# The first MLP's leaky ReLU on three engines, without the linear product, and its output product three slots behind

## The chip, the cores and the metric

One NeuronCore of a Trainium2 chip runs the kernel. The metric is the device time of one execution in microseconds (us).

## The reference

All sizes and steps, with x running through one attention and two MLPs:

```python
# attention: q (12288 x 128), kv pooled 4x4 to 768 keys, then @ w_sr; k = v
s = (q @ k.T) / sqrt(128); a = exp(s - max); a /= a.sum() + 1e-9; x = a @ v
# first MLP: 128 -> 2048 -> 128
h = x @ w_in;  g = maximum(0.01 * h, h);  x = g @ w_out
# second MLP: 128 -> 2048 -> 128
h = x @ w_in2; g = where(h >= 1, h, where(h <= -1, 0, (h + 1)**2 / 4)); out = g @ w_out2
```

## The kernel before

The 12,288 tokens are cut into 24 blocks of 512 (TB). Everything is kept transposed: channels on the partitions, tokens along the free axis. The hidden 2,048 channels of each MLP are 16 chunks (FC) of 128, one per slot `s`.

Every matmul operand is split into a high part (fp32r) and the low part that is left, so each product is three matmuls of 512 columns: low weight with high data, high weight with high data, high weight with low data (`product`, L484 to L488). This is why each intermediate needs a high part (a copy, by ScalarE) and a low part (a subtraction, by VectorE or GpSimd).

Each engine has its own program, and semaphores tie them together. All programs go through iterations `j`, each of 16 slots. Iteration j works on three blocks at once: the first MLP of block j, the second MLP of block j-1 (and the last chunks of block j-2), and the attention of block j+1. Iteration 0 has no second MLP, iteration 23 has no attention, iteration 24 has the second MLP alone. Before iteration 0 stand the pooling of kv, the splitting of the weights and block 0's attention.

Names used below, with the line where each is issued:

- `mlp1_in(s)`: the hidden product of the first MLP, chunk s, into one of two PSUM banks `h1`. It waits until the chunk two back has been read. `mlp1_out(s)`: the output product of chunk s, added up in `sum1`; it is issued LAG1 slots behind.
- `mlp2_in(s)`, `mlp2_out(s)`: the same of the second MLP (`h2`, `sum2`), LAG2 = 3 slots behind.
- g1 high: ScalarE, L342, a ReLU from PSUM. g1 low: VectorE, L458, `max(h, 0) - high`.
- ramp: ScalarE, L351, into `g2`. bend: VectorE, L445, `min(g2, 1) * g2`, both inputs in SBUF. above: VectorE, L451, `max(h, g2)`. g2_high: ScalarE, L329. g2_low: GpSimd, L267.
- attention of the next block: `score` (4 of them, slots 0, 2, 4, 6), row maximum (L377), exponential (L283, slots 1, 3, 5, 7), normalisation (L288, slots 2, 4, 6, 8), transposes (L507, slots 9 to 14) with high and low part (L293, L390), `values` (slots 10 to 15), attended high and low part (L297, L395).
- x2 high and low part (L369, L477): the first MLP's sum as input of the second.

The leaky ReLU is written as a sum: `max(0.01 h, h) = 0.99 (relu(h) + h * 0.01 / 0.99)`. The second term is linear in x, so its path through both weights is one 128 x 128 matrix `lin`, made once before iteration 0 from 16 matmuls (L553), and applied to the block by one product at slot 2 of each iteration, ahead of the first `mlp1_out`:

```python
def mlp1_out(s):
    fs = slice(s * P, (s + 1) * P)
    if s == 0:
        product(sum1, lin_hi[:], lin_lo[:], x_hi[:], x_lo[:], True, False)
    pe.wait_ge(g1_split, j * FC + s + 1)
```

GpSimd's queue, in order: the identity, the low part of the queries, the split of w1_out, four quarters of w1_in's low part (each waits for ScalarE, which does the second to fourth inside slots 0 to 2 of iteration 0), the splits of w2_in and w2_out, and then its iterations.

The lines that a program prints:

## Time and profile before

| | |
|---|---|
| device time, median of 3 runs | 1396.45 us (1395.6 to 1396.55) |
| the profiled execution's span, first to last instruction | 1394.2 us |
| TensorE busy | 1368.8 us, 98% of the span |
| VectorE busy | 1035.5 us, 74% |
| ScalarE busy | 950.9 us, 68% |
| GpSimd busy | 563.7 us, 40% |

The trace gives the span; the execution's own time around it is not recorded apart, and the median of the runs is 2.3 us above the span. Times in the trace count from the span's start. A matmul's row lasts longer than the distance to the next, since matmuls overlap; distances between starts tell the pace. A row's time before the engine's name is its start, then its duration. Where a row ends in brackets, the engine sat idle that long, until the operation named there was done.

### The profile page before, as it was taken

Reading aid. Unit: us, or ns where it says so; the run is one execution under the profiler, and the core shown is the slowest. Engines: PE = TensorE matmul, PEld = TensorE weight load, DVE = VectorE, ACT = ScalarE, POOL = GpSimd, SP = SyncE. Lnnn points to the kernel's source line nnn. Section 1 sums busy time; section 2 is a strip of 40 time slices with the busy share of each in tenths; the row PEclk is TensorE's granted clock in tenths of the full one; section 3 lists DMA queues with packets and bytes.
Section 4 is the critical chain, followed back from the end, with each engine's and each line's share of the span. In section 5 each row is a group of like instructions: output and inputs, shape, how many; then the busy total and the mean of one; then the engine's idle time right before and its main releaser. Section 6 shows DMA issues by size and latency. Waiting matters only on the chain.

```text
span 1394.2 us, 21088 instructions
## 1 busy us (share of the span) xinstructions
PE 1368.8 (98%) x6320; PEld 1115.3 (80%) x6320; DVE 1035.5 (74%) x1660; ACT 950.9 (68%) x1695; POOL 563.7 (40%) x424
## 2 busy tenths in 40 slices
PE   5999999999999999999999999999999999999997
PEld 4788888888888888888888888888888888888884
DVE  6577777777777777777787777777877777777777
ACT  3676776766767667677676676776766767667665
POOL 2534344334334344343434434344334334344346
PEclk9999999999999999999999999999999999999999
DMA  8000000000000000000000000000000000000000
GB/s 348 16 0 8 9 15 8 8 15 8 8 8 8 15 8 8 15 2 13 8 8 15 8 8 8 8 15 8 8 15 8 8 8 8 15 0 9 8 1 16
DMA packets 9525, 24.44 MB, mean 18 GB/s; under 512 B 1057, under 2 KB 1185, under 8 KB 8865
## 3 DMA queue, kind: packets, MB, share of 16 engines
q1 hardware_dynamic: 9504, 24.19, 4.9%
q8 instruction: 11, 0.18, 0.1%
q14 instruction: 10, 0.07, 0.0%
HBM read 17.89 MB, written 6.29 MB: 17 GB/s over the span
## 4 chain that ended last, share of the span: by engine, by line
PE 95%; DVE 3%; DMA 1%; ACT 0%; issue 0%; SPq 0%; POOL 0%; POOLq 0%
PE sums L487 13%; PE sums L488 13%; PE sums L486 13%; PE hidden L486 13%; PE hidden L488 13%; PE hidden L487 13%; PE attn L488 5%; PE attn L486 5%; PE attn L487 5%; PE attn L507 4%; DVE stage L445 1%; DVE stage L451 1%; DVE probs L411 1%; DMA stage<-kvT 1%; DVE neg_max L377 0%; PE hidden L507 0%
## 5 line engine op out<-in xcount | busy, mean ns | idle before, releaser
L267 POOL TENSOR_TENSOR g_lo<-stage,g_hi 128x512 fp32r<-128x512 f32 x384 | 508.6, 1324 | 790.4 <-ACT g_hi L329 790.3
L458 DVE SCALAR_TENSOR_TENSOR g_lo<-hidden,g_hi 128x512 fp32r<-128x512 f32 x384 | 265.4, 691 | 265.8 <-ACT g_hi L342 264.3
L342 ACT ACTIVATE g_hi<-hidden 128x512 fp32r<-128x512 f32 x384 | 230.0, 599 | 281.1 <-PE hidden L488 271.8
L445 DVE SCALAR_TENSOR_TENSOR stage<-stage 128x512 f32<-128x512 f32 x384 | 270.9, 705 | 23.1 <-ACT stage L351 21.4
L351 ACT ACTIVATE stage<-hidden 128x512 f32<-128x512 f32 x384 | 230.1, 599 | 74.1 <-PE hidden L488 42.6
L451 DVE TENSOR_TENSOR stage<-hidden,stage 128x512 f32<-128x512 f32 x384 | 265.5, 691 | 13.1
L329 ACT ACTIVATE g_hi<-stage 128x512 fp32r<-128x512 f32 x384 | 242.1, 630 | 31.7 <-DVE stage L451 31.6
L486 PE MATMUL sums<-g_hi,w2o_lo 128*128 128x512 f32 x384 | 152.8, 398 | 4.4 <-POOL g_lo L267 2.8
L486 PE MATMUL hidden<-x_hi,w1i_lo 128*128 128x512 f32 x384 | 152.0, 396 | 1.5 <-DVE x_lo L395 1.5
L486 PE MATMUL sums<-g_hi,w1o_lo 128*128 128x512 f32 x384 | 153.3, 399 | 0.0
L488 PE MATMUL sums<-g_lo,w2o_hi 128*128 128x512 f32 x384 | 151.7, 395 | 0.0
L487 PE MATMUL hidden<-x_hi,w1i_hi 128*128 128x512 f32 x384 | 151.7, 395 | 0.0
L488 PE MATMUL hidden<-x_lo,w2i_hi 128*128 128x512 f32 x384 | 151.7, 395 | 0.0
L486 PE MATMUL hidden<-x_hi,w2i_lo 128*128 128x512 f32 x384 | 151.5, 395 | 0.1
L487 PE MATMUL sums<-g_hi,w2o_hi 128*128 128x512 f32 x384 | 151.6, 395 | 0.0
L487 PE MATMUL sums<-g_hi,w1o_hi 128*128 128x512 f32 x384 | 151.5, 395 | 0.0
L488 PE MATMUL hidden<-x_lo,w1i_hi 128*128 128x512 f32 x384 | 151.2, 394 | 0.0
L488 PE MATMUL sums<-g_lo,w1o_hi 128*128 128x512 f32 x384 | 151.2, 394 | 0.0
L487 PE MATMUL hidden<-x_hi,w2i_hi 128*128 128x512 f32 x384 | 150.7, 392 | 0.0
L486 PEld LDWEIGHTS sums<-g_hi,w2o_lo 128*128 128x128 f32 x384 | 72.2, 188 | 26.1 <-POOL g_lo L267 9.2
L390 DVE TENSOR_TENSOR pT_lo<-attn,pT_hi 128x512 fp32r<-128x512 f32 x135 | 91.8, 680 | 0.1
L486 PEld LDWEIGHTS hidden<-x_hi,w1i_lo 128*128 128x128 f32 x384 | 72.3, 188 | 19.0 <-issue 1.9
(107 smaller groups left out, 2090.2 us busy)
## 6 DMA issues: line engine op xcount, KB each, us to landing
q_raw<-qT SPq DMA_DIRECT2D x24, 256.0 KB, 2.7
stage<-kvT SPq DMA_DIRECT2D x12, 512.0 KB, 8.8
outT<-stage SPq DMA_DIRECT2D x24, 256.0 KB, 2.0
stage<-w_out SPq DMA_DIRECT2D x2, 1024.0 KB, 14.1
...
```

Source lines behind the costliest of these rows:

```text
L267: nc.gpsimd.tensor_tensor(g2_lo[s % RING][:], g2[s % RING], g2_hi[s % RING][:].bitcast(F32), ALU.subtract).then_inc(g2_split, 1)
L329: nc.scalar.activation(g2_hi[s % RING][:], g2[s % RING], ACT.Copy).then_inc(g2_hi_done, 1)
L342: nc.scalar.activation(g1_hi[s % RING][:], h1[s % HBANKS], ACT.Relu).then_inc(g1_hi_done, 1)
L351: nc.scalar.activation(g2[s % RING], h2_banks(do)[s % len(h2_banks(do))], ACT.Relu, bias=0.5, scale=0.5).then_inc(ramp_done, 1)
L390: nc.vector.tensor_tensor(pT_lo[k][:], probsT_of(a, k), pT_hi[k][:].bitcast(F32), ALU.subtract).then_inc(pT_split, 1)
L445: nc.vector.scalar_tensor_tensor(g2[s % RING], g2[s % RING], 1.0, g2[s % RING], ALU.min, ALU.mult).then_inc(bent_done, 1)
L451: nc.vector.tensor_tensor(g2[s % RING], h2_banks(do)[s % len(h2_banks(do))], g2[s % RING], ALU.max).then_inc(g2_done, 1)
L458: nc.vector.scalar_tensor_tensor(g1_lo[s % RING][:], h1[s % HBANKS], 0.0, g1_hi[s % RING][:].bitcast(F32), ALU.max, ALU.subtract).then_inc ...
L486: nc.tensor.matmul(out, w_lo, m_hi, start=start, stop=False)
L487: nc.tensor.matmul(out, w_hi, m_hi, start=False, stop=False)
L488: return nc.tensor.matmul(out, w_hi, m_lo, start=False, stop=stop)
L507: last = nc.tensor.transpose(probsT_of(a, k)[:, t * P:(t + 1) * P], probs[t][:, k * P:(k + 1) * P], ident[:])
```

## The change

The linear term goes, and with it the matrix `lin`, its product in each block, and the load of the transposed w1_in. The leaky ReLU is taken as it stands: ScalarE writes `0.01 h` (leak) from PSUM to a ring of four SBUF buffers `g1` (in the space of a staging buffer that has become free), VectorE takes the maximum with `h` in place, ScalarE copies the high part one slot later (`g1_high(s - 1)`), and GpSimd subtracts for the low part. In GpSimd's queue this subtraction of chunk s stands ahead of that of the second MLP's chunk s. The bank of `h1` is free after the maximum (`g1_done`). `mlp1_out` goes from two slots behind to three: three of them stand after slot 15 in place of two. Its first one starts the sum and waits for the previous block's sum to be read. The scaling by 0.99 goes from the x2 parts. Before iteration 0 TensorE waits for all four exponentials.

```diff
@@ -38,7 +38,7 @@
 SUB = TB // P
 RING = 4
 HBANKS = 2
-LAG1, LAG2 = 2, 3
+LAG1, LAG2 = 3, 3
 QUARTERS = 4
 HALVES = 2
 
...
@@ -78,7 +78,7 @@
         iteration(j, parts(j))
 
 
-def build(nc, qT, kvT, w_sr, w1_in, w1_inT, w1_out, w2_in, w2_out, outT):
+def build(nc, qT, kvT, w_sr, w1_in, w1_out, w2_in, w2_out, outT):
     ctx = ExitStack()
     with ctx:
         def sb(name, cols, dt=F32):
...
@@ -90,12 +90,11 @@
 
         ident = sb("ident", P)
         stage = [sb(f"stage{k}", FF) for k in range(KC)]
-        W1O_RAW, W1IT_RAW, W1I_RAW, W2I_RAW, W2O_RAW = stage[:5]
+        W1O_RAW, W1I_RAW, W2I_RAW, W2O_RAW = stage[0], *stage[2:5]
         w1i_hi, w1i_lo = sb("w1i_hi", FF, F32R), sb("w1i_lo", FF, F32R)
         w1o_hi, w1o_lo = sb("w1o_hi", FF, F32R), sb("w1o_lo", FF, F32R)
         w2i_hi, w2i_lo = sb("w2i_hi", FF, F32R), sb("w2i_lo", FF, F32R)
         w2o_hi, w2o_lo = sb("w2o_hi", FF, F32R), sb("w2o_lo", FF, F32R)
-        lin_hi, lin_lo = sb("lin_hi", P, F32R), sb("lin_lo", P, F32R)
         kT_hi, kT_lo = sb("kT_hi", KEYS, F32R), sb("kT_lo", KEYS, F32R)
         v_hi, v_lo = sb("v_hi", KEYS, F32R), sb("v_lo", KEYS, F32R)
 
...
@@ -109,6 +108,7 @@
         pT_lo = [sb(f"pT_lo{k}", TB, F32R) for k in range(KC)]
         x_hi, x_lo = sb("x_hi", TB, F32R), sb("x_lo", TB, F32R)
         x2_hi, x2_lo = sb("x2_hi", TB, F32R), sb("x2_lo", TB, F32R)
+        g1 = [stage[1][:, n * TB:(n + 1) * TB] for n in range(RING)]
         g1_hi = [sb(f"g1_hi{n}", TB, F32R) for n in range(RING)]
         g1_lo = [sb(f"g1_lo{n}", TB, F32R) for n in range(RING)]
         g2 = [stage[KC - 1][:, n * TB:(n + 1) * TB] for n in range(RING)]
...
@@ -171,7 +170,6 @@
         w2i_hi_done, w2o_hi_done = sem("w2i_hi_done"), sem("w2o_hi_done")
         w1i_split, w1o_split = sem("w1i_split"), sem("w1o_split")
         w2i_split, w2o_split = sem("w2i_split"), sem("w2o_split")
-        lin_ready, lin_hi_done, lin_split = sem("lin_ready"), sem("lin_hi_done"), sem("lin_split")
 
         q_loaded = sem("q_loaded")
         q_hi_done, q_split = sem("q_hi_done"), sem("q_split")
...
@@ -185,8 +183,8 @@
 
         probsT_ready, pT_hi_done, pT_split = sem("probsT_ready"), sem("pT_hi_done"), sem("pT_split")
 
-        h1_ready, g1_hi_done, g1_split, g1_used = (
-            sem("h1_ready"), sem("g1_hi_done"), sem("g1_split"), sem("g1_used"))
+        h1_ready, leak_done, g1_done, g1_hi_done, g1_split, g1_used = (
+            sem("h1_ready"), sem("leak_done"), sem("g1_done"), sem("g1_hi_done"), sem("g1_split"), sem("g1_used"))
         h2_ready, ramp_done, bent_done, g2_done, g2_hi_done, g2_split, g2_used = (
             sem("h2_ready"), sem("ramp_done"), sem("bent_done"), sem("g2_done"),
             sem("g2_hi_done"), sem("g2_split"), sem("g2_used"))
...
@@ -209,7 +207,6 @@
                 sp.dma_start(raw, dram).then_inc(loaded, 16)
 
             load_weight(0, w1_out, w1o_loaded)
-            load_weight(1, w1_inT, w1it_loaded)
             load_weight(2, w1_in, w1i_loaded)
             sp.wait_ge(q_split, 1)
             sp.dma_start(q_raw[:], qT[:, TB:2 * TB]).then_inc(q_loaded, 16)
...
@@ -261,6 +258,12 @@
 
             def iteration(j, do):
                 for s in range(FC):
+                    if do.mlp1:
+                        n = j * FC + s
+                        pool.wait_ge(g1_hi_done, n + 1)
+                        nc.gpsimd.tensor_tensor(g1_lo[s % RING][:], g1[s % RING],
+                                                g1_hi[s % RING][:].bitcast(F32),
+                                                ALU.subtract).then_inc(g1_split, 1)
                     if do.mlp2:
                         n = (j - 1) * FC + s
                         pool.wait_ge(g2_hi_done, n + 1)
...
@@ -308,8 +311,6 @@
             normalise(0, 0)
             for k in range(KC):
                 transposed_hi(0, k)
-            act.wait_ge(lin_ready, 1)
-            nc.scalar.activation(lin_hi[:], lin_sum, ACT.Copy, scale=LEAK / (1.0 - LEAK)).then_inc(lin_hi_done, 1)
             split_queries(1)
 
             def split_w1_in(n):
...
@@ -321,6 +322,13 @@
             attended_hi(0)
 
             def iteration(j, do):
+                def g1_high(s):
+                    n = j * FC + s
+                    act.wait_ge(g1_done, n + 1)
+                    if not (isinstance(j, int) and n < RING):
+                        act.wait_ge(g1_used, n - RING + 1)
+                    nc.scalar.activation(g1_hi[s % RING][:], g1[s % RING], ACT.Copy).then_inc(g1_hi_done, 1)
+
                 def g2_high(s):
                     n = (j - 1) * FC + s
                     act.wait_ge(g2_done, n + 1)
...
@@ -338,8 +346,10 @@
                         n = j * FC + s
                         act.wait_ge(h1_ready, n + 1)
                         if not (isinstance(j, int) and n < RING):
-                            act.wait_ge(g1_used, n - RING + 1)
-                        nc.scalar.activation(g1_hi[s % RING][:], h1[s % HBANKS], ACT.Relu).then_inc(g1_hi_done, 1)
+                            act.wait_ge(g1_split, n - RING + 1)
+                        nc.scalar.activation(g1[s % RING], h1[s % HBANKS], ACT.Copy, scale=LEAK).then_inc(leak_done, 1)
+                        if s > 0:
+                            g1_high(s - 1)
                     if do.attend and s == FC - 1:
                         attended_hi(j + 1)
                     if do.mlp2:
...
@@ -362,11 +372,13 @@
                         split_queries(j + 2)
                     if isinstance(j, int) and j == 0 and s < QUARTERS - 1:
                         split_w1_in(s + 1)
+                if do.mlp1:
+                    g1_high(FC - 1)
                 if do.mlp2:
                     g2_high(FC - 1)
                 if do.mlp1:
                     act.wait_ge(g1_used, FC * (j + 1))
-                    nc.scalar.activation(x2_hi[:], sum1, ACT.Copy, scale=1.0 - LEAK).then_inc(x2_hi_done, 1)
+                    nc.scalar.activation(x2_hi[:], sum1, ACT.Copy).then_inc(x2_hi_done, 1)
 
             every_iteration(act, iteration)
 
...
@@ -433,9 +445,6 @@
             normalise(SUB - 1)
             for k in range(KC):
                 transposed_lo(0, k)
-            dve.wait_ge(lin_hi_done, 1)
-            nc.vector.scalar_tensor_tensor(lin_lo[:], lin_sum, LEAK / (1.0 - LEAK), lin_hi[:].bitcast(F32),
-                                           ALU.mult, ALU.subtract).then_inc(lin_split, 1)
             attended_lo(0)
 
             def iteration(j, do):
...
@@ -454,10 +463,9 @@
                 for s in range(FC):
                     if do.mlp1:
 
-                        dve.wait_ge(g1_hi_done, j * FC + s + 1)
-                        nc.vector.scalar_tensor_tensor(g1_lo[s % RING][:], h1[s % HBANKS], 0.0,
-                                                       g1_hi[s % RING][:].bitcast(F32),
-                                                       ALU.max, ALU.subtract).then_inc(g1_split, 1)
+                        dve.wait_ge(leak_done, j * FC + s + 1)
+                        nc.vector.tensor_tensor(g1[s % RING], h1[s % HBANKS], g1[s % RING],
+                                                ALU.max).then_inc(g1_done, 1)
                     if do.attend and s == 0:
                         row_max(j + 1, 0)
                     if do.attend and s == FC - 1:
...
@@ -474,8 +482,7 @@
                         transposed_lo(j + 1, TRANSPOSE_SLOT[s])
                 if do.mlp1:
                     dve.wait_ge(x2_hi_done, j + 1)
-                    nc.vector.scalar_tensor_tensor(x2_lo[:], sum1, 1.0 - LEAK, x2_hi[:].bitcast(F32),
-                                            ALU.mult, ALU.subtract).then_inc(x2_split, 1)
+                    nc.vector.tensor_tensor(x2_lo[:], sum1, x2_hi[:].bitcast(F32), ALU.subtract).then_inc(x2_split, 1)
 
             every_iteration(dve, iteration)
 
...
@@ -545,20 +552,12 @@
                 first_score(t, TB, KEYS).then_inc(scores_ready, 1)
 
 
-            pe.wait_ge(w1o_loaded, 16)
-            pe.wait_ge(w1it_loaded, 16)
-            pe.wait_ge(exp_done, 1)
-            for f in range(FC):
-                fs = slice(f * P, (f + 1) * P)
-                last = nc.tensor.matmul(lin_sum, W1IT_RAW[:, fs], W1O_RAW[:, fs], start=(f == 0), stop=(f == FC - 1))
-            last.then_inc(lin_ready, 1)
+            pe.wait_ge(exp_done, SUB)
             pe.wait_ge(ident_ready, 1)
             for k in range(KC):
                 transpose(0, k)
             for k in range(KC):
                 values(0, k)
-            pe.wait_ge(lin_split, 1)
-            pe.wait_ge(w1o_split, 1)
 
             def iteration(j, do):
                 def mlp1_in(s):
...
@@ -569,17 +568,19 @@
                     if s == 0:
                         pe.wait_ge(x_split, j + 1)
                     if not (isinstance(j, int) and n < HBANKS):
-                        pe.wait_ge(g1_split, n - HBANKS + 1)
+                        pe.wait_ge(g1_done, n - HBANKS + 1)
                     product(h1[s % HBANKS], w1i_hi[:, fs], w1i_lo[:, fs], x_hi[:], x_lo[:], True,
                             True).then_inc(h1_ready, 1)
 
                 def mlp1_out(s):
                     fs = slice(s * P, (s + 1) * P)
-                    if s == 0:
-                        product(sum1, lin_hi[:], lin_lo[:], x_hi[:], x_lo[:], True, False)
+                    if isinstance(j, int) and j == 0 and s == 0:
+                        pe.wait_ge(w1o_split, 1)
+                    if s == 0 and not (isinstance(j, int) and j == 0):
+                        pe.wait_ge(x2_split, j)
                     pe.wait_ge(g1_split, j * FC + s + 1)
                     product(sum1, w1o_hi[:, fs], w1o_lo[:, fs], g1_hi[s % RING][:], g1_lo[s % RING][:],
-                                   False, s == FC - 1).then_inc(g1_used, 1)
+                                   s == 0, s == FC - 1).then_inc(g1_used, 1)
 
                 def mlp2_in(s):
                     fs = slice(s * P, (s + 1) * P)
...
@@ -653,7 +654,6 @@
         "kvT": windows.transpose(4, 0, 2, 1, 3).reshape(P, TOKENS),
         "w_sr": w_sr,
         "w1_in": moe_w_in,
-        "w1_inT": moe_w_in.reshape(P, FC, P).transpose(2, 1, 0),
         "w1_out": moe_w_out.reshape(FC, P, P).transpose(1, 0, 2),
         "w2_in": moe2_w_in,
         "w2_out": moe2_w_out.reshape(FC, P, P).transpose(1, 0, 2),
```

## Rows read from the trace of the kernel before

**Rows 1.** The page, part 1: busy time of each engine.

```profile
PE 1368.8 (98%) x6320; PEld 1115.3 (80%) x6320; DVE 1035.5 (74%) x1660; ACT 950.9 (68%) x1695; POOL 563.7 (40%) x424
```

**Rows 2.** The page, part 4: chain of waits, by engine.

```profile
PE 95%; DVE 3%; DMA 1%; ACT 0%; issue 0%; SPq 0%; POOL 0%; POOLq 0%
```

**Rows 3.** Windows: stretch, length, then PE, PEld, DVE, ACT, POOL busy, clock, DMA.

```profile
692.79:749.12 56.33, 56.33 (x263) 46.15 (x261) 42.18 (x68) 39.44 (x71) 22.37 (x17) 1.00 0.03 9
```

**Rows 4.** Groups of instructions: busy us, mean ns, idle before.

```profile
L267 POOL TENSOR_TENSOR g_lo<-stage,g_hi 128x512 fp32r<-128x512 f32 x384 | 508.6, 1324 | 790.4 <-ACT g_hi L329 790.3
L445 DVE SCALAR_TENSOR_TENSOR stage<-stage 128x512 f32<-128x512 f32 x384 | 270.9, 705 | 23.1 <-ACT stage L351 21.4
L451 DVE TENSOR_TENSOR stage<-hidden,stage 128x512 f32<-128x512 f32 x384 | 265.5, 691 | 13.1
...
L488 PE MATMUL sums<-x_lo,lin_hi 128*128 128x512 f32 x24 | 9.7, 403 | 0.0
```

**Rows 5.** Timeline, TensorE, slot 2 of a steady iteration.

```profile
700.44 0.39 PE L486 MATMUL sums<-x_hi,lin_lo 128*128 128x512 f32 x1
...
701.15 0.40 PE L486 MATMUL sums<-g_hi,w1o_lo 128*128 128x512 f32 x1
```

**Rows 6.** Timeline, TensorE, the first transposes after the linear weight's matmuls.

```profile
31.86 0.41 PE L507 MATMUL hidden<-ident,probs 128*128 128x128 f32 x2 [0.47 <-DVE probs L423]
```

**Rows 7.** Timeline, ScalarE, a stretch in which it never waits.

```profile
698.09 0.90 ACT L283 ACTIVATE probs<-attn,neg_max 128x768 f32<-128x768 f32 x1
...
698.96 0.63 ACT L329 ACTIVATE g_hi<-stage 128x512 fp32r<-128x512 f32 x1
699.48 0.60 ACT L342 ACTIVATE g_hi<-hidden 128x512 fp32r<-128x512 f32 x1
699.96 0.60 ACT L351 ACTIVATE stage<-hidden 128x512 f32<-128x512 f32 x1
700.44 0.65 ACT L329 ACTIVATE g_hi<-stage 128x512 fp32r<-128x512 f32 x1
```

**Rows 8.** Timeline, GpSimd and VectorE, last iteration.

```profile
1370.07 1.39 POOL L267 TENSOR_TENSOR g_lo<-stage,g_hi 128x512 fp32r<-128x512 f32 x1 [0.31 <-ACT g_hi L329]
...
1370.95 1.06 DVE L445 SCALAR_TENSOR_TENSOR stage<-stage 128x512 f32<-128x512 f32 x1
```

**Rows 9.** Timeline, GpSimd and VectorE, slot 2 of a steady iteration.

```profile
700.97 0.68 DVE L445 SCALAR_TENSOR_TENSOR stage<-stage 128x512 f32<-128x512 f32 x1
...
701.16 1.64 POOL L267 TENSOR_TENSOR g_lo<-stage,g_hi 128x512 fp32r<-128x512 f32 x1 [0.20 <-ACT g_hi L329]
```

**Rows 10.** Timeline, GpSimd, iteration 0.

```profile
47.00 1.30 POOL L257 TENSOR_TENSOR w1i_lo<-stage,w1i_hi 128x512 fp32r<-128x512 f32 x1 [0.53 <-ACT w1i_hi L318]
48.25 1.91 POOL L247 CAST w2i_hi<-stage 128x2048 fp32r<-128x2048 f32 x1
...
56.79 4.62 POOL L249 TENSOR_TENSOR w2o_lo<-stage,w2o_hi 128x2048 fp32r<-128x2048 f32 x1
```

**Rows 11.** Timeline, GpSimd and TensorE, last iteration: a product that waits for its low part.

```profile
1383.71 1.37 POOL L267 TENSOR_TENSOR g_lo<-stage,g_hi 128x512 fp32r<-128x512 f32 x1 [0.32 <-ACT g_hi L329]
...
1385.13 0.50 PE L486 MATMUL sums<-g_hi,w2o_lo 128*128 128x512 f32 x1 [0.73 <-POOL g_lo L267]
...
1385.47 0.39 PE L487 MATMUL sums<-g_hi,w2o_hi 128*128 128x512 f32 x1
```

**Rows 12.** Timeline, VectorE and TensorE, slots 9 and 10 of a steady iteration.

```profile
724.93 0.68 DVE L390 TENSOR_TENSOR pT_lo<-attn,pT_hi 128x512 fp32r<-128x512 f32 x1
...
725.98 0.60 PE L507 MATMUL attn<-ident,probs 128*128 128x128 f32 x4
```

**Rows 13.** Timeline, TensorE: iteration 0's first output product, iteration 1's first matmul.

```profile
45.35 0.39 PE L486 MATMUL sums<-g_hi,w1o_lo 128*128 128x512 f32 x1
...
74.83 0.39 PE L486 MATMUL hidden<-x_hi,w1i_lo 128*128 128x512 f32 x1
```

**Rows 14.** Timeline, TensorE, its first dense stretch.

```profile
21.62 0.63 PE L488 MATMUL attn<-kT_lo,q_hi 128*128 128x512 f32 x1
```

3 lines of the change are left out of this document (1 added, 2 removed).

## The prediction

> **What bounds the kernel now.** I read the page first: TensorE is busy 98% of the span [rows 1], and the chain of waits is TensorE for 95% [rows 2]. The chain also says that VectorE (3%) and DMA (1%) matter only at the start. Then I cut one block's iteration out of the steady loop, from its first matmul to that of the next block: 56.33 us, TensorE busy all of it, VectorE 42.18, ScalarE 39.44, GpSimd 22.37 [rows 3]. So every matmul removed counts in full, as long as the three helper engines still deliver in time. They are not the bound by their sums; the question is when, in each slot, the last of them is done. The groups of instructions give what each operation takes [rows 4], the timelines how closely two follow each other.
>
> **Gain.** The linear product is three matmuls per block, x24 [rows 4]. The first starts at 700.44 and the next product at 701.15 [rows 5]: 0.70 us, which is also what every other product costs. Over 24 blocks that is -16.8 us. At the start, the 16 matmuls that build the linear weight vanish too, but the transposes behind them waited 0.47 us more, for VectorE's last normalisation [rows 6]: worth 0. The 1 MB load that goes is no wait of anything; 0.
>
> **What is added.** Per chunk: ScalarE gets one more copy. Back to back, ScalarE starts an instruction 0.48 us after one that reads PSUM, 0.52 after one that reads SBUF, 0.87 after an exponential [rows 7]. So +0.52 us, 16 times a block: 8.3, giving 47.7 of 55.6 us. VectorE swaps a 0.69 us operation for one that should take the same, as the maximum of L451 does [rows 4]: 0. GpSimd gets a second subtraction of 1.32 us mean [rows 4], 21.1 us more a block: 43.5 of 55.6. By sums all of it fits. By order it does not, at four places.
>
> **The lock.** "Bend" (L445) reads SBUF twice. In the last iteration it takes 1.06 instead of 0.69 us whenever it starts inside a GpSimd subtraction: started 1370.95, while GpSimd runs 1370.07 to 1371.46, it ends at 1372.01, 0.55 after GpSimd [rows 8]. The other way round, a subtraction that starts at 701.16 inside a bend that ends at 701.65 takes 1.64 and ends 1.15 after the bend [rows 9]. So either waits for the other. The maxima, with one input in PSUM, stay at 0.69. This goes into the sum as "bend ends 0.55 after the GpSimd operation that it meets". The new order makes the meeting the rule: ScalarE finishes g1_high(s-1) about 0.5 us ahead of the ramp of s, so GpSimd has started when bend(s) comes up, and bend loses up to 1.1 us in nearly every slot, with everything behind it on VectorE (the maximum, the row maxima, the transposed low parts).
>
> The Trainium skill, "SBUF — State Buffer", section "Who interferes with whom", states this as a rule: a VectorE instruction with two SBUF inputs and a GpSimd one that reads SBUF block each other whole, by order of start. The traces agree. With the rule the sum below is 1492; a reader who doubts it gets the 1446 of the third rival.
>
> **Steady block, walked slot by slot** (T is the start of the slot's first matmul; a product 0.70; ScalarE starts 0.89 after the first matmul of a three-matmul product; a consumer starts 0.03 to 0.07 us after its producer's end).
>
> *Slot 15.* PE wants: mlp1_in T, values 0.70, mlp2_in 1.40, then first-MLP output 12, second-MLP output 12, first-MLP outputs 13, 14, 15, the last due at T+5.4 with the 0.50 us that values(5) is late (below). ScalarE: leak(15) 0.89, g1_high(14) 1.37, the attended copy 2.1, ramp(15) 2.8, g2_high(14) 3.3, g1_high(15) 3.8 to 4.4. GpSimd: g1_lo(14), then g2_lo(14) 4.0 to 5.3, then g1_lo(15), which starts 1.25 after the one before it (as 47.00 to 48.25 [rows 10]) and ends at 6.5. TensorE starts a matmul 0.05 after the GpSimd end (1385.08 to 1385.13) and its next comes 0.34 later instead of 0.23 [rows 11], so a late operand costs its lateness plus 0.16. Stall: **1.29 us**. It cannot hide: nothing of the next block stands ahead of it in TensorE's queue. Before, VectorE did this low part without a queue.
>
> *Slots 9 and 10.* pT_lo(0) was ready at 725.61 and the next transpose went at 725.98 [rows 12]: 0.37 spare. Now, from T of slot 9: normalise(3) and g1_high push ScalarE, ramp(9) ends at 2.65, g1_lo(8) runs 2.60 to 3.89, bend(9) ends 4.45, its maximum 5.17, pT_lo(0) 5.77. The transpose was due at 4.61. Stall **1.32 us**. In slots 11 to 14 (0.70 longer) the same chain leaves 0, 0.09, 0 and 0.28: **0.37**. In slot 15 values(5) needs pT_lo(5) at T+0.70, and it ends at 1.04: **0.50**.
>
> *Slots 2 and 4.* A score product waits for the exponential two slots back in ScalarE's order, which comes 0.3 us later for the added copy, and in slot 4 also behind a row maximum held up by bend: **0.11 + 0.37**.
>
> Sum of stalls 3.96; less the 0.70 gained and 0.06 of rounding, a block takes 56.33 + 3.20 = 59.5 us. Blocks 1 to 22 have this shape: **+70.4 us**.
>
> **Block 0.** GpSimd's queue has the splits of the second MLP's weights ahead of its loop: the last ends at 61.41 [rows 10]. They start behind w1i_lo, which waits for ScalarE, 1.05 us later with two more ScalarE copies ahead: 62.5. Only then comes g1_lo(0), done at 63.7; the first output product, which started at 45.35 [rows 13], can start at 63.76. Behind it in TensorE's queue is everything. From 45.35 to block 1's first matmul at 74.83 were 29.48 us [rows 13]; one input product now stands ahead of the wait (-0.70), and I add 0.11 restart, 0.9 for ScalarE's four slots with exponentials, 1.03 for g1_lo(15) at the end. That puts block 1 at 94.6, **+19.8 us** (the linear product's 0.70 is in it).
>
> **Block 23** has no attention, so slots of four products, 2.79 us. GpSimd and bend together need 1.29 + 0.55 + 1.15 - 0.04 = 2.95 a slot. The slack of two slots hides half of the 2.6 us that builds up; the last g1_lo is about 3.6 late: -0.7 + 1.0 + 3.6 = **+3.9**. Block 24 runs the second MLP alone, unchanged: 0.
>
> **Clock.** A matmul of the first dense stretch took 0.63 us [rows 14], against 0.39 later [rows 13]. After 18 idle us in block 0 TensorE may fall to that pace again for a while: 0 to 3 us, I take **+1.5**.
>
> Sum: 70.4 + 19.8 + 3.9 + 1.5 = 95.6. The profiled execution's span is 1394.2; that makes 1489.8. The median shown is 2.3 us above the span, so **1492 us**. All costs are from rows but two: the new maximum with g1 in SBUF and h1 in PSUM (0.69, as L451; if the lock held it too, +0.5 a chunk, in the heavy rival) and the leak copy (0.60 as the ramp; nothing cheaper or dearer stands near it).
>
> **Rivals.**
> 1. *The extra slot of lag covers the loop* (the other side). Mechanism: GpSimd runs g1_lo(15) ahead of need, and bend slips between its operations. For it: by sums GpSimd has 12 us spare in a block. Against it: g2_lo(14) stands ahead of g1_lo(15) and waits for g2_high(14), which waits for ramp(15). The loop would give -16.1 and block 0 +19.8: 1400. It turns faster only when block 0's wait is under 16.1 us, at best 1380. Chance 0.06, of which 0.03 faster.
> 2. *Lateness adds up* (heavy). If both GpSimd operations get ahead of bend in the transposed slots, as in slot 10, each of five loses 0.3 more, and the row maxima push in the same way: +1.5 a block, 33 in all, 1525; up to 1550 if the new maximum is held too. Chance 0.18.
> 3. *No meeting of GpSimd and bend in most slots.* Then stalls are 0.11, 0.2, 0.3, 0.06 and 1.3, 2.0 a block: 22 x 1.3 = 28, block 0 19.8, block 23 1, together 49: 1446. For it: spans on GpSimd are rough and bend could slip ahead. Chance 0.16.
>
> My forecast has 0.60. Its own range is 1465 to 1515. The 8-in-10 range takes in rival 3 and most of rival 2: 1440 to 1530. Within 0.2% (2.8 us, about what a measurement of this kernel can tell from no change) only part of rival 1 falls: faster 0.03, same 0.02, slower 0.95.
>
> **What the profile after would show.** TensorE's wait for g_lo on GpSimd as the largest; one of 17 to 19 us before 65 us; some 1.3 us once a block before the last first-MLP output; about 1.3 us before the second transposed chunk of each block; a mean for bend of 1.1 to 1.4 us (now 0.705); a block of 59 to 60 us; the linear rows gone. Wrong would be: GpSimd's 18 us wait absent (my reading of its queue), a mean for bend near 0.7 (the lock), or a block under 56.3 us (the walk).

## The result and the profile after

The changed kernel takes **1499.86 us** (median of 4 runs, 1498.54 to 1501.44) against 1396.31 of the kernel before: ratio 1.0742, 95% interval 1.0727 to 1.0757. It is slower by 103.5 us. The profiled execution took 1501.4, with a span of 1499.7; it is 1.6 us above the median, so its rows stand for a little more than the typical run. Part of that lies at the start: its first exponential begins at 27.44, while in four other profiles of kernels with the same start it begins between 26.23 and 27.00.

The page of the changed kernel, parts 1, 2 and 4, for [rows 1] and [rows 2]:

```profile
PE 1390.9 (93%) x6216; PEld 1087.7 (73%) x6216; DVE 1232.9 (82%) x1659; ACT 1109.5 (74%) x2078; POOL 1114.6 (74%) x808
...
PEclk9799999999999999999999999999999999999999
...
POOL 57%; issue 29%; PE 6%; DVE 5%; ACT 2%; POOLq 1%; DMA 0%; SPq 0%; ACTq 0%
```

No engine is at its limit, and yet the end depends on GpSimd: a chain that was 95% TensorE now passes through GpSimd for 57% (29% is "issue", time in which the engine waited for nothing that the profile shows). TensorE's granted clock dips in the second slice.

The groups of GpSimd's two subtractions and of bend, for [rows 4] (L270 is the old L267, L264 is new, L454 is the old L445):

```profile
L270 POOL TENSOR_TENSOR g_lo<-stage,g_hi 128x512 fp32r<-128x512 f32 x384 | 579.1, 1508 | 116.9 <-ACT g_hi L337 116.8
L264 POOL TENSOR_TENSOR g_lo<-stage,g_hi 128x512 fp32r<-128x512 f32 x384 | 496.8, 1294 | 225.6 <-ACT g_hi L330 221.2
L454 DVE SCALAR_TENSOR_TENSOR stage<-stage 128x512 f32<-128x512 f32 x384 | 496.5, 1293 | 52.5 <-ACT stage L361 50.1
```

Bend has gone from 705 to 1293 ns in the mean, and g2's subtraction from 1324 to 1508. The maxima, which read one input from PSUM, take 687 ns (the new one) and 691 ns (the old one, unmoved).

One steady block, from its first matmul to the next block's, for [rows 3]. First the length, then PE, PEld, DVE, ACT and POOL busy, clock, DMA:

```profile
755.73:815.32 59.59, 57.10 (x259) 44.89 (x258) 50.49 (x68) 45.96 (x86) 45.30 (x34) 1.00 0.03 9
```

The low part of x2 comes once a block, so its starts mark the blocks. VectorE's timeline of the changed kernel:

```profile
101.75 0.69 DVE L485 TENSOR_TENSOR x_lo<-sums,x_hi 128x512 fp32r<-128x512 f32 x1 [3.09 <-ACT x_hi L381]
160.58 0.69 DVE L485 TENSOR_TENSOR x_lo<-sums,x_hi 128x512 fp32r<-128x512 f32 x1 [3.36 <-ACT x_hi L381]
...
1412.09 0.69 DVE L485 TENSOR_TENSOR x_lo<-sums,x_hi 128x512 fp32r<-128x512 f32 x1 [3.36 <-ACT x_hi L381]
1463.24 0.69 DVE L485 TENSOR_TENSOR x_lo<-sums,x_hi 128x512 fp32r<-128x512 f32 x1 [3.52 <-ACT x_hi L381]
```

and of the kernel before:

```profile
75.66 0.69 DVE L477 SCALAR_TENSOR_TENSOR x_lo<-sums,x_hi 128x512 fp32r<-128x512 f32 x1 [1.40 <-ACT x_hi L369]
130.36 0.69 DVE L477 SCALAR_TENSOR_TENSOR x_lo<-sums,x_hi 128x512 fp32r<-128x512 f32 x1 [1.37 <-ACT x_hi L369]
...
1313.22 0.69 DVE L477 SCALAR_TENSOR_TENSOR x_lo<-sums,x_hi 128x512 fp32r<-128x512 f32 x1 [1.38 <-ACT x_hi L369]
1358.82 0.69 DVE L477 SCALAR_TENSOR_TENSOR x_lo<-sums,x_hi 128x512 fp32r<-128x512 f32 x1 [1.37 <-ACT x_hi L369]
```

The 105.5 us by which the span grew (1394.2 to 1499.7) fall into: block 0, 101.75 - 75.66 = **+26.1**; block 1, 58.83 - 54.70 = +4.1; blocks 2 to 22, 21 x (59.60 - 56.33) = **+68.7**; block 23, 51.15 - 45.60 = **+5.5**; what follows, +1.1.

Why a block is longer. TensorE's largest waits in the changed kernel, for the start of a matmul (PE) or of a weight load (PEld), which overlaps the matmul before. Columns: us in total, times, the longest:

```profile
PEld attn L514 <- DVE pT_lo L402: 54.4, 88, 1.5
...
PE sums L493 <- POOL g_lo L264: 44.4, 27, 18.0
PEld sums L493 <- POOL g_lo L264: 37.8, 26, 2.4
...
PE attn L514 <- DVE pT_lo L402: 24.0, 22, 1.1
PEld attn L493 <- ACT probs L286: 19.5, 44, 1.2
```

Inside the block of the window above, the starts of the matmuls leave five gaps of over 0.2 us beyond the usual distance: 0.27 before the third score product (768.71), 1.25 before the second transposed chunk (789.33), 0.23 before the last transposed chunk (805.36), 0.39 before the last values product (809.04) and 1.19 before the last output product (814.52). They sum to 3.33 us. Another 0.64 is the slower restart behind each (0.11, [rows 11]) and smaller ones: 3.97 in all, less the 0.70 that was gained, gives 3.27. Two of the gaps in TensorE's timeline:

```profile
789.33 0.66 PE L514 MATMUL attn<-ident,probs 128*128 128x128 f32 x4 [1.09 <-DVE pT_lo L402]
...
814.52 0.51 PE L493 MATMUL sums<-g_hi,w1o_lo 128*128 128x512 f32 x1 [1.02 <-POOL g_lo L264]
```

and what stood in their way, on GpSimd's timeline:

```profile
783.14 1.30 POOL L264 TENSOR_TENSOR g_lo<-stage,g_hi 128x512 fp32r<-128x512 f32 x1
784.39 1.76 POOL L270 TENSOR_TENSOR g_lo<-stage,g_hi 128x512 fp32r<-128x512 f32 x1
...
811.94 1.30 POOL L270 TENSOR_TENSOR g_lo<-stage,g_hi 128x512 fp32r<-128x512 f32 x1 [0.59 <-ACT g_hi L337]
813.20 1.26 POOL L264 TENSOR_TENSOR g_lo<-stage,g_hi 128x512 fp32r<-128x512 f32 x1
```

and VectorE's:

```profile
783.34 1.65 DVE L454 SCALAR_TENSOR_TENSOR stage<-stage 128x512 f32<-128x512 f32 x1
785.03 0.69 DVE L460 TENSOR_TENSOR stage<-hidden,stage 128x512 f32<-128x512 f32 x1
```

Bend starts at 783.34 inside GpSimd's subtraction (783.14 to 784.44) and ends at 784.99, 0.55 after it: the wait of [rows 8]. Of all 384 bends 337 start inside a GpSimd subtraction, and each of these ends 0.54 to 0.56 us after it. GpSimd's next, begun at 784.39 inside bend, ends at 786.15, 1.16 after bend, as in [rows 9]. At the block's end g2_lo(14) (811.94) stands ahead of g1_lo(15) (813.20 to 814.46), and TensorE starts the last output product 0.06 us later.

Block 0, for [rows 6], [rows 10] and [rows 13]. TensorE's timeline:

```profile
32.86 3.65 PE L514 MATMUL hidden<-ident,probs 128*128 128x128 f32 x16 [4.69 <-DVE probs L435]
...
44.16 0.47 PE L493 MATMUL hidden<-x_hi,w1i_lo 128*128 128x512 f32 x1 [1.51 <-DVE x_lo L407]
...
67.27 0.76 PE L493 MATMUL sums<-g_hi,w1o_lo 128*128 128x512 f32 x1 [17.97 <-POOL g_lo L264]
```

and GpSimd's:

```profile
61.41 4.49 POOL L246 TENSOR_TENSOR w2o_lo<-stage,w2o_hi 128x2048 fp32r<-128x2048 f32 x1
65.86 3.73 POOL L264 TENSOR_TENSOR g_lo<-stage,g_hi 128x512 fp32r<-128x512 f32 x3
```

The 18 us wait is there: the subtractions of the first MLP begin when the last weight split is done (65.86), and the first output product follows at 67.27, 21.9 us after that of before. But the first row was not foreseen: with the linear weight's matmuls gone, TensorE idles 4.69 us ahead of the transposes and then does 16 of them in 3.65 us. Windows of that start, columns as above:

```profile
28.00:32.00 4.00, 0.16 (x2) 0.00 (x0) 3.86 (x13) 3.90 (x9) 2.15 (x1) 0.98 0.51 213
32.00:36.00 4.00, 3.14 (x15) 3.17 (x16) 1.90 (x4) 1.51 (x3) 0.00 (x0) 0.50 0.00 0
```

Granted clock 0.50, the 1.2 GHz level, right behind a stretch in which TensorE did nearly nothing.

### The profile page after: what moved, and what is told of

Its sections match the earlier page's. It is cut to its first block, busy times and chain, and to the rows that moved or that the text cites. A ratio compares the mean times of both kernels' runs of the same rounds, so it can differ in the third digit from the quotient of the medians.

```text
span 1499.7 us, 22367 instructions
## 1 busy us (share of the span) xinstructions
PE 1390.9 (93%) x6216; PEld 1087.7 (73%) x6216; DVE 1232.9 (82%) x1659; ACT 1109.5 (74%) x2078; POOL 1114.6 (74%) x808
## 4 chain that ended last, share of the span: by engine, by line
POOL 57%; issue 29%; PE 6%; DVE 5%; ACT 2%; POOLq 1%; DMA 0%; SPq 0%; ACTq 0%
POOL g_lo L270 29%; POOL g_lo L264 25%; DVE stage L454 2%; POOL q_lo L238 1%; DVE stage L460 1%; PE sums L493 1%; PE hidden L493 1%; DVE probs L423 1%; PE hidden L495 1%; PE hidden L494 1%; PE sums L495 1%; PE sums L494 1%; PE attn L493 1%; ACT g_hi L330 1%; PE attn L494 0%
## 5 line engine op out<-in xcount | busy, mean ns | idle before, releaser
L270 POOL TENSOR_TENSOR g_lo<-stage,g_hi 128x512 fp32r<-128x512 f32 x384 | 579.1, 1508 | 116.9 <-ACT g_hi L337 116.8
L264 POOL TENSOR_TENSOR g_lo<-stage,g_hi 128x512 fp32r<-128x512 f32 x384 | 496.8, 1294 | 225.6 <-ACT g_hi L330 221.2
L454 DVE SCALAR_TENSOR_TENSOR stage<-stage 128x512 f32<-128x512 f32 x384 | 496.5, 1293 | 52.5 <-ACT stage L361 50.1
L350 ACT ACTIVATE stage<-hidden 128x512 f32<-128x512 f32 x384 | 230.0, 599 | 202.5 <-PE hidden L495 196.9
L467 DVE TENSOR_TENSOR stage<-hidden,stage 128x512 f32<-128x512 f32 x384 | 263.8, 687 | 77.2 <-ACT stage L350 75.2
L460 DVE TENSOR_TENSOR stage<-hidden,stage 128x512 f32<-128x512 f32 x384 | 265.5, 691 | 13.2
L337 ACT ACTIVATE g_hi<-stage 128x512 fp32r<-128x512 f32 x384 | 244.0, 635 | 31.4 <-DVE stage L460 31.3
L361 ACT ACTIVATE stage<-hidden 128x512 f32<-128x512 f32 x384 | 229.3, 597 | 46.0 <-PE hidden L495 43.7
L330 ACT ACTIVATE g_hi<-stage 128x512 fp32r<-128x512 f32 x384 | 241.6, 629 | 0.0
L493 PE MATMUL sums<-g_hi,w1o_lo 128*128 128x512 f32 x384 | 156.8, 408 | 44.4 <-POOL g_lo L264 44.4
L493 PEld LDWEIGHTS sums<-g_hi,w1o_lo 128*128 128x128 f32 x384 | 72.6, 189 | 68.8 <-POOL g_lo L264 37.8
```

What stands on the lines that cost most here:

```text
L264: nc.gpsimd.tensor_tensor(g1_lo[s % RING][:], g1[s % RING], g1_hi[s % RING][:].bitcast(F32), ALU.subtract).then_inc(g1_split, 1)
L270: nc.gpsimd.tensor_tensor(g2_lo[s % RING][:], g2[s % RING], g2_hi[s % RING][:].bitcast(F32), ALU.subtract).then_inc(g2_split, 1)
L330: nc.scalar.activation(g1_hi[s % RING][:], g1[s % RING], ACT.Copy).then_inc(g1_hi_done, 1)
L337: nc.scalar.activation(g2_hi[s % RING][:], g2[s % RING], ACT.Copy).then_inc(g2_hi_done, 1)
L350: nc.scalar.activation(g1[s % RING], h1[s % HBANKS], ACT.Copy, scale=LEAK).then_inc(leak_done, 1)
L361: nc.scalar.activation(g2[s % RING], h2_banks(do)[s % len(h2_banks(do))], ACT.Relu, bias=0.5, scale=0.5).then_inc(ramp_done, 1)
```

## The experiments

Each edit is in the changed kernel unless "before" is said. Line numbers in rows of experiments are shifted by the edits. Ratios are to the kernel before.

**Bend with one input from SBUF.** Its first input is h's PSUM bank, and nothing else moves. It computes `min(h, 1)` times the ramp, another curve than the reference.

```diff
-nc.vector.scalar_tensor_tensor(g2[s % RING], g2[s % RING], 1.0, g2[s % RING], ALU.min, ALU.mult)
+nc.vector.scalar_tensor_tensor(g2[s % RING], h2_banks(do)[s % len(h2_banks(do))], 1.0, g2[s % RING], ALU.min, ALU.mult)
```

> The changed kernel, with one input of bend taken from PSUM: min(h, 1) * ramp in place of min(ramp, 1) * ramp, so that bend reads SBUF once (its values differ from the reference's). Theory of the lock (bend and GpSimd's subtraction wait for each other when bend reads SBUF twice): bend's mean falls from 1.29 us to 0.69, GpSimd's from 1.29 and 1.51 to 1.29 and 1.29, the steady block loses the wait of the second transposed chunk (1.3 to about 0.3), that of the values (0.4 to 0.1) and some of the scores', and falls from 59.6 to about 57.6 us; the time to about 1450 (1440 to 1460). Rival, ScalarE's added copy is what makes everything late: bend gets shorter but the block stays within 0.3 us of 59.6, the time above 1490. In both, the last output product of a block still waits for GpSimd, about 1.3 us.

Measured: 1446.56 us, ratio 1.0359 (1.0342 to 1.0376): 53.3 us less than the changed kernel. A steady block takes 57.65 us, 1.95 less. Its groups:

```profile
L454 DVE SCALAR_TENSOR_TENSOR stage<-hidden,stage 128x512 f32<-128x512 f32 x384 | 265.1, 690 | 113.0 <-ACT stage L361 113.0
...
L270 POOL TENSOR_TENSOR g_lo<-stage,g_hi 128x512 fp32r<-128x512 f32 x384 | 498.1, 1297 | 86.6 <-ACT g_hi L337 83.5
```

Both prolonged groups are back at their undisturbed size, and TensorE's matmul wait for pT_lo ahead of a transpose is gone. Its wait for GpSimd's g1_lo stays at 42.9 us: that one is of another kind. Most of the score products' waits stay as well: slots 2 and 4 of a block are still 0.44 us longer than in the kernel before without its linear product (the run below), after 0.52 in the changed kernel. The Trainium skill ("SBUF — State Buffer", "Who interferes with whom") names two SBUF inputs as the condition; taking one away does here what its rule says.

**The same edit in the kernel before.**

> The kernel before with the same edit of bend (one input from PSUM, values differ from the reference's). Theory of the lock: there bend hardly meets GpSimd (mean 0.705), but for the last iteration, where it took 1.06; that iteration may lose up to 16 x 0.3 = 5 us, the steady block stays at 56.33, the time 1391 to 1396.5. Rival, the edit makes the kernel faster for another reason than the lock: the steady block moves.

Measured: 1391.4 us, ratio 0.9964 (0.9949 to 0.9978). The steady block stays at 56.33; the whole gain of 5 us is in the last iteration. So bend meets GpSimd in the old order too, but costs time only there, where a slot holds no more than the second MLP's two products. Against this kernel, and not against 1396.3, the changed kernel with the same edit is to be measured: it is 55.2 us behind.

**GpSimd does g1_lo(15) before g2_lo(14).** ScalarE's g1_high(15) goes ahead of ramp(15), or GpSimd would wait for it.

```diff
-                    if do.mlp2:
-                        n = (j - 1) * FC + s
...
+                    if do.mlp2 and s != FC - 2:
+                        for c in ((s,) if s < FC - 1 else (s - 1, s)):
...
+                    if do.mlp1 and s == FC - 1:
+                        g1_high(s)
```

> The changed kernel, where only the end of each block is reordered: ScalarE makes the high part of chunk 15 ahead of the ramp of chunk 15, and GpSimd takes the low part of chunk 15 ahead of the second MLP's of chunk 14. Theory of the queue (the last output product waits for g1_lo(15), which stands behind g2_lo(14)): that wait of about 1.3 us a block goes, 59.6 becomes 58.3 us, in all 23 x 1.3 = 30 us, and some 1 to 2 us in block 23 more: about 1468 (1462 to 1474). Rival, GpSimd has too much to do as a whole: the wait only moves into the next block, the block stays above 59.2, the time above 1490.

Measured: 1469.56 us, ratio 1.0527 (1.051 to 1.0545): 30.3 us less than the changed kernel, 1.30 per steady block (58.30). TensorE's matmul waits for g1_lo, 27 before, are down to three in block 0 and two at the end of block 23 (1.56 and 0.29 us); those for pT_lo are untouched:

```profile
PE attn L514 <- DVE pT_lo L402: 23.8, 22, 1.1
PE sums L493 <- POOL g_lo L264: 20.4, 5, 18.0
```

**The splits of w2_in and w2_out in quarters**, one behind each odd slot of iteration 0 in GpSimd's queue.

```diff
-            split_weight(W2I_RAW, w2i_hi, w2i_lo, w2i_loaded, w2i_hi_done, w2i_split)
-            split_weight(W2O_RAW, w2o_hi, w2o_lo, w2o_loaded, w2o_hi_done, w2o_split)
...
+                    if isinstance(j, int) and j == 0 and s % 2 == 1:
+                        k = s // 2
+                        if k < QUARTERS:
+                            split_quarter(W2I_RAW, w2i_hi, w2i_lo, w2i_loaded, w2i_hi_done, w2i_split, k)
```

> The changed kernel, where GpSimd splits the second MLP's weights in quarters between its subtractions of iteration 0 in place of all ahead of them. Theory of block 0: TensorE's wait of 18 us before 68 us goes; GpSimd still has 13 us more to do in iteration 0 than it had room for by perhaps 3 to 5, which comes back at the start of block 1; net -11 to -17 us, 1483 to 1489, steady block unchanged at 59.6. Rival, the 18 us are hidden in the end because block 1 would wait for the second MLP's weights anyway: 1497 or more.

Measured: 1489.21 us, ratio 1.0666 (1.0649 to 1.0684), 10.7 us less, at the edge of what was expected (1489, 11 us). The 18 us wait is 5.2, and x2's first low part starts at 88.67 in place of 101.75, 13.1 earlier, of which the span kept 12.6. (The medians differ by less than the spans, for the reason given with the result.) Block 0 is still 13.0 us later than before: GpSimd has the same work to do inside it; that this is the reason is argued, not tested.

**16 filler matmuls** ahead of block 0's transposes, into an unused part of the attention bank, in the place of the linear weight's.

```diff
+            for f in range(FC):
+                nc.tensor.matmul(attn[:, TB:TB + P], W1O_RAW[:, fs], W1O_RAW[:, fs], start=(f == 0), stop=(f == FC - 1))
             pe.wait_ge(exp_done, SUB)
```

> The changed kernel with 16 matmuls of no use (weights by weights into a free part of PSUM) where the linear weight's stood, ahead of block 0's transposes. Theory of the clock (without them TensorE waits 5.4 us for the probabilities and its first transposes and values run at half pace: 16 transposes took 3.65 us in the changed kernel, 1.94 before): the transposes take 1.9 to 2.0 us again, block 0's first hidden product comes 2.5 to 3 us earlier, the time falls by 2 to 3 us. Rival, the later start of block 0 (44.16 against 40.37) comes from the loads alone: no change, within 1 us.

Measured: 1497.31 us, ratio 1.0721 (1.0707 to 1.0736), 2.6 us less. TensorE's timeline has the transposes at full pace again:

```profile
32.51 1.94 PE L514 MATMUL hidden<-ident,probs 128*128 128x128 f32 x16 [0.48 <-DVE probs L435]
```

The first hidden matmul comes at 41.01 in place of 44.16 (before: 40.37). Counted from the first exponential, which takes the executions' own difference out, it comes 13.93 us later here, 13.93 before, and 16.26 to 16.72 in the five profiles of kernels that have neither the linear weight's matmuls nor the fillers. So the clock costs 2.3 to 2.8 us here, and the fillers bring back all of it.

**LAG1 back to 2**, in the changed kernel.

> The changed kernel with LAG1 back at 2. Theory (the last output product of a block is fixed by when GpSimd delivers, whatever was issued before it; inside the block the low parts are more than a slot early): one product less stands behind slot 15, its wait is 0.7 longer, the end is the same: block 59.6 +- 0.3, time 1496 to 1506. Rival, the third slot is what keeps the body running: with two slots the outputs wait in most slots, the block takes 61 us or more, the time above 1525.

Measured: 1507.71 us, ratio 1.0795 (1.0778 to 1.0812), a block of 59.85. The third slot is worth 7.9 us, more than expected (1496 to 1506 for this run), and hides a small part of what GpSimd's place in the path costs.

**The kernel before without its linear product** (three matmuls a block less, all else kept).

```diff
-                    if s == 0:
-                        product(sum1, lin_hi[:], lin_lo[:], x_hi[:], x_lo[:], True, False)
...
-                                   False, s == FC - 1).then_inc(g1_used, 1)
+                                   s == 0, s == FC - 1).then_inc(g1_used, 1)
```

It leaves out the negative side of the leaky ReLU, and it still loads and multiplies the linear weight's matrices at the start.

> The kernel before with the linear product left out of every block (the negative side of the leaky ReLU is missing, the linear weight is still made). This is the gain alone. Theory: 24 x 0.70 = 16.8 us, block 55.63, time 1379.5 (1378.5 to 1381). Rival, ScalarE or VectorE are so near the bound that less comes back: above 1384.

Measured: 1380.18 us, ratio 0.9885 (0.987 to 0.99). A block takes 55.62 (0.71 less). The gain by itself is 16.2 us.

**The four edits at once** (bend, order, quarters, fillers).

> The changed kernel with the four single edits at once: bend with one input from PSUM (values differ from the reference's), the last first-MLP chunk first, the second MLP's weights in pieces, the filler matmuls. Theory (four causes, each its own): their single gains add up, 53.3 + 30.3 + 10.7 + 2.6 = 96.9, time 1403 (1396 to 1408), block 56.4 (57.65 less 1.3). Rival, they overlap, so that taking one away uncovers another wait: less than 85 in all, above 1415.

Measured: 1403.23 us, ratio 1.0048 (1.0033 to 1.0064). The single gains are 53.3 + 30.3 + 10.7 + 2.6 = 96.9, and 1499.9 - 96.9 = 1403.0: they add up. What is left of waits, for the weight loads:

```profile
PEld attn L503 <- ACT probs L296: 17.0, 44, 0.7
...
PEld attn L524 <- DVE pT_lo L412: 9.0, 22, 0.4
PEld attn L503 <- DVE pT_lo L412: 5.8, 23, 0.3
```

The block takes 56.35. Slot by slot, against the kernel before without its linear product, the 0.70 goes to the score products of slots 2 and 4, which wait for ScalarE's exponential (0.45), to the transposed chunk of slot 10 (0.20) and to slot 15 (0.09). Block 0 is still 11.9 us later than before. Of that the execution itself began 1.1 us later; TensorE's waits for g1_lo are 5.2, 1.9 and 0.3 us, and behind the first of them the granted clock is 0.50 up to 56.8, for 5.0 us, which costs half of that. The bend of this version is not the reference's; the kernel before with the same bend takes 1391.4, so that what is left of the loss is 11.8 us.

### Four attempts at a better kernel

**Clamp and square.** The curve is `max(h, square(0.5 clamp(h, -1, 1) + 0.5))`: VectorE clamps from PSUM (one input), ScalarE squares, VectorE takes the maximum one slot later. The weights' splits are spread over three engines, the fillers are in, and in GpSimd's queue g2_lo(s-1) stands ahead of g1_lo(s).

```diff
+nc.vector.tensor_scalar(g2[s % RING], h2_banks(do)[s % len(h2_banks(do))], 1.0, -1.0,
+                        ALU.min, ALU.max).then_inc(ramp_done, 1)
...
+nc.scalar.activation(g2[s % RING], g2[s % RING], ACT.Square, bias=0.5,
+                     scale=0.5).then_inc(bent_done, 1)
```

> A version that computes the reference whole: the changed kernel's first MLP, but the second MLP's activation as clamp (VectorE, from PSUM) then square (ScalarE) then maximum one slot later (VectorE), so that no VectorE instruction of the loop reads SBUF twice; the high part of the first MLP's chunk in its own slot; low parts of the second MLP one slot later in GpSimd's queue, behind nothing that the last first-MLP product needs; the second MLP's weights split in quarters by GpSimd, ScalarE and VectorE during iteration 0; filler matmuls as in the experiment above. Theory (lock, queue order, weight splits and clock are all of the loss, ScalarE's 47.7 us of work fit in 55.6): block 55.6 to 56.2, no wait of 18 us, time 1375 to 1392, faster than before. Rival, ScalarE with four instructions and the exponentials in one slot is a bound of its own: block 57 us or more, time above 1405.

Measured: 1488.14 us, ratio 1.0659 (1.0642 to 1.0675). A miss, 96 us above what was expected, on the side of the rival. TensorE's waits:

```profile
PE attn L512 <- ACT probs L296: 29.9, 44, 1.2
PE attn L533 <- ACT probs L301: 23.8, 23, 3.3
```

The score products and transposes wait for ScalarE's exponentials and normalisations. In slots 1 to 8 a slot takes 3.32 us in the mean, against 3.00 in the kernel before without its linear product, where TensorE does not wait (one output product taken off, for the third slot of lag). Each slot now passes VectorE, ScalarE, VectorE, ScalarE, and ScalarE's queue holds the exponential inside that circle: with the lock gone, another engine's order is the bound, as the next attempt tests.

**The same with the exponential and normalisation right behind leak, and g2_high last in its slot.**

> The clamp and square version with another order on ScalarE: exponential and normalisation right behind the leak, high part of the second MLP's previous chunk last in the slot. Theory of the loop (before, maximum of s-1 on VectorE, its high part, the exponential, the high part of chunk s, the square of s and the maximum of s stood in one circle of about 3.3 us a slot in slots 1 to 8, against 3.31 us of TensorE work, and the score waited for the exponential): the circle no longer holds the exponential, the scores' waits of 3 us a block go to under 1, block 59.25 becomes 55.8 to 57.2, time 1390 to 1430. Rival, ScalarE's sum in slots 1 to 8 is the bound, not its order: block stays above 58.5, time above 1470.

Measured: 1511.4 us, ratio 1.0823 (1.0807 to 1.084). A miss, 81 us above the top of what was expected. Slots 1 to 8 fell to 3.14 us each, so ScalarE's order had been the bound there, but g2_high(14) came later, g2_lo(14) with it, and g1_lo(15) stood behind. TensorE's timeline:

```profile
749.49 0.50 PE L512 MATMUL sums<-g_hi,w1o_lo 128*128 128x512 f32 x1 [2.28 <-POOL g_lo L276]
```

That wait then cost more than itself. Windows, columns as above:

```profile
744.00:748.00 4.00, 3.22 (x14) 2.26 (x13) 2.38 (x4) 2.79 (x5) 2.34 (x3) 1.00 0.00 0
750.00:754.00 4.00, 4.00 (x13) 3.27 (x13) 1.71 (x3) 1.82 (x3) 0.79 (x2) 0.57 0.00 0
754.00:758.00 4.00, 4.00 (x18) 3.22 (x18) 2.66 (x5) 2.00 (x5) 1.19 (x1) 1.00 0.00 0
```

The granted clock fell to 0.57 in the four us behind the wait. The same wait, 2.27 or 2.28 us, ends each of blocks 1 to 22, and the clock fell behind 15 of the 22: a block that begins with the fall takes 60.3 to 60.8 us, one without it 59.1 to 59.5 (the mean is 60.3).

**GpSimd's g1_lo(s) ahead of g2_lo(s-1)**, on top of it, and w1_in's quarters in slots 0, 3 and 6.

> The version of the exponentials first, computing the reference whole, with two edits of order on GpSimd: in each slot the low part of the first MLP's chunk goes ahead of the second MLP's previous chunk, and the low quarters of w1_in are spread over slots 0, 3 and 6 of iteration 0. Theory of the queue (in that version the last output product of each block waited 3.1 us for g1_lo(15) behind g2_lo(14), and TensorE then ran at half pace for about 3 us more): both go, block 60.7 becomes 55.9 to 57, block 0 ends 5 us earlier, time 1388 to 1412, so about the kernel before. Rival, the wait moves on to g2_lo, now the later one, or to ScalarE's copy of the output: block above 58.5, time above 1450.

Measured: 1424.17 us, ratio 1.0196 (1.0182 to 1.021). The steady block (56.7) is as expected, 3.6 us under the mean of the attempt before; the time is above the expectation's range. Against the kernel before it loses 8.1 us in block 0, 8.5 in blocks 1 to 22, 4.9 in block 23 and 6.6 behind it. The score products no longer wait in slots 2 and 4 (0.03 us together). The largest wait left in the steady block is for ScalarE's copy of the second MLP's sum, and slot 3, where it stands, is 1.05 us too long:

```profile
716.82 0.50 PE L516 MATMUL sums<-g_hi,w2o_lo 128*128 128x512 f32 x1 [0.79 <-ACT stage L358]
```

**The kernel before with clamp and square in its last iteration alone.** ScalarE has no attention work there.

```diff
+                    if do.mlp2 and not do.mlp1:
+                        act.wait_ge(ramp_done, (j - 1) * FC + s + 1)
+                        nc.scalar.activation(g2[s % RING], g2[s % RING], ACT.Square, bias=0.5,
+                                             scale=0.5).then_inc(bent_done, 1)
...
+                        nc.vector.tensor_scalar(g2[s % RING], h2_banks(do)[s % len(h2_banks(do))], 1.0, -1.0,
+                                                ALU.min, ALU.max).then_inc(ramp_done, 1)
+                        if s > 0:
+                            above(s - 1)
```

> The kernel before, computing the reference whole, with one edit: in the last iteration, where only the second MLP runs, clamp on VectorE from PSUM and square on ScalarE in place of ramp and bend. Theory of the lock: the last iteration's slot falls from 1.71 us to 1.39, as when bend read SBUF once; time 1391.5 (1390.5 to 1393). Rival, the circle VectorE, ScalarE, GpSimd is the bound there, not the lock: 1395 or more.

Measured: **1391.76 us**, ratio 0.9968 (0.9956 to 0.998). It beats both kernels of this study. VectorE's timeline in the last iteration:

```profile
1366.55 0.69 DVE L473 TENSOR_SCALAR stage<-hidden 128x512 f32<-128x512 f32 x1 [0.52 <-PE hidden L502]
1367.16 0.68 DVE L455 TENSOR_TENSOR stage<-hidden,stage 128x512 f32<-128x512 f32 x1
```

and GpSimd's, which overlaps it:

```profile
1365.91 3.98 POOL L267 TENSOR_TENSOR g_lo<-stage,g_hi 128x512 fp32r<-128x512 f32 x3 [0.24 <-ACT g_hi L329]
```

No VectorE instruction there is longer than 0.69 us, where [rows 8] had 1.06. From x2's last low part to the end it is 30.6 us in place of 35.3.

## Why the prediction was right, and where its sizes were off

The main path was the predicted one, and the time (1499.9 against 1492) fell inside its own range of 1465 to 1515. It was not reached by errors that cancel: every part of the sum came out a little above its forecast (blocks 1 to 22 72.8 for 70.4, block 0 26.1 for 21.3, block 23 5.5 for 3.9, the rest 1.1 for 0). Point by point:

- **Gain.** -16.8 forecast, -16.2 measured by itself. The load that went brought no earlier start: the first exponential begins at 26.15 to 27.10 in four profiles with it, at 26.23 to 27.44 in five without. The two costs without a row came as taken: the new maximum 687 ns, the leak copy 599.
- **The lock.** Forecast: bend's mean 1.1 to 1.4 us, by meeting GpSimd in most slots. Measured 1.29, and taking the second SBUF input away gives 53.3 us. The third rival (no meeting in most slots, 1446) is what the first experiment builds: 1446.6. Block and block 23 agree with it (+1.32 for the 1.3, +1.1 for the 1), but that the sum does is partly luck: block 0 was 25.1 later than before in place of 19.8, and the last iteration, which the rival left out, 5.1 shorter.
- **GpSimd's order at a block's end.** Forecast 1.29, measured 1.19; the order alone gives 30.3 us.
- **Steady block.** Forecast 59.5, measured 59.60. Each slot's length, from its first hidden matmul to the next slot's, less that of the kernel without the linear product (0.70 moved from slot 2 to slot 15 for the third slot of lag), mean over the steady blocks: slots 2 and 4 0.52 for the forecast 0.48, slot 10 1.30 for 1.32, slots 11 to 14 0.33 for 0.37, slot 15 1.80 for 1.29 + 0.50. The walk was right term by term. In block 1 slot 4 is another 0.7 longer. The heavy rival (+1.5 a block) did not come.
- **Block 0.** Forecast 19.8, with 1.5 for the clock 21.3; measured 26.1. The wait for the weight splits came as read (18.0 us, over at 67.27 against 63.76). The step that failed is the start: *"the transposes behind them waited 0.47 us more ... worth 0"*. The linear weight's matmuls were cover of another kind: they kept TensorE's clock at 2.4 GHz. Without them the first hidden matmul came 3.8 us later; 1.0 of it had arisen before the exponentials and is the profiled execution's own (the same start begins them between 26.23 and 27.44, the old one at 26.44), and 2.8 is half pace with what hangs on it. The fillers took 3.15 us of it back at that point and 2.6 of the time. Behind the 18 us wait the clock was at half again, from 67.27 to about 72.8, some 2.7 us in place of the 1.5 taken. With 3.8, the term that was put at 0, and 2.7 the forecast's 19.8 comes to 26.3.
- **Block 23.** Forecast +3.9, measured +5.5. The pair of GpSimd and bend has the pace forecast, 2.96 us a slot for 2.95, as VectorE's timeline shows:

```profile
1421.79 1.72 DVE L454 SCALAR_TENSOR_TENSOR stage<-stage 128x512 f32<-128x512 f32 x1
1424.74 1.72 DVE L454 SCALAR_TENSOR_TENSOR stage<-stage 128x512 f32<-128x512 f32 x1
```

  The step that failed is *"the slack of two slots hides half"* (half of 2.6 would be 1.3; the sum took 1.0). TensorE itself goes at 2.91 to 2.97 a slot from slot 4 on (its first hidden matmuls at 1420.62, 1423.53, 1426.48, up to 1453.13), against 2.79 before: the hidden products wait for their banks, which are free after the operation behind bend. The waits of that stretch (1418 to 1456):

```profile
PEld hidden L493 <- DVE stage L460: 4.0, 12, 0.3
```

  That is 12 slots with 2.0 us more than before in all. The last two output products wait 1.55 and 1.94 more (3.9 with the restarts), where the forecast had 3.6, and from the last one to x2's low part it is 0.3 longer: -0.7 + 2.0 + 3.9 + 0.3 = 5.5.
- **What follows block 23.** Forecast 0, measured +1.1. The forecast had no clock term here. Behind the two waits TensorE's clock falls once more:

```profile
1462.00:1465.40 3.40, 3.40 (x10) 2.63 (x9) 0.69 (x1) 0.60 (x1) 0.57 (x1) 0.50 0.00 0
```

  From x2's last low part (1463.24) to 1465.4 that is 2.2 us at half pace, 1.1 us lost. In the run in which GpSimd does g1_lo(15) first, the clock stays at 1.00 there, and the stretch to the end is 35.3 us, as in the kernel before (here 36.4).
- **Rival 1** (the lag covers it) is out: the third slot is worth 7.9 us, against 83.6 that the lock and the order cost together. It could not help more because the last chunk of a block has no other product behind which its lateness could hide, whatever the lag.

Even with all four causes removed (1403.2) the change is not ahead of the kernel before (1396.3, or 1391.4 with the same bend): block 0 still ends 11.9 us later, and each block gives back the 0.70 us that the linear product had cost. That GpSimd's second subtraction crowds block 0, and that ScalarE's extra copy makes the exponentials late, is read from the waits; no run takes either away by itself. In favour of the second: the third attempt, with the exponentials earlier in ScalarE's queue, has no such wait, though its second activation differs as well.

Open: why slot 4 of block 1 is 0.7 us longer than in the other blocks; the losses of the third attempt in block 0, in block 23 and behind it, of which its trace shows only that the granted clock is 0.50 from 1380.0 to 1383.4, from 1390.2 to 1393.6 and from 1414.1 to the end; and whether any order of the changed kernel gets under 1391.8 us. Three attempts did not. The version that beats both kernels leaves the change out.
